# Paired query transposes, alternating GpSimd sums, and the row maximum placed by ScalarE in a one-core attention and soft-MoE kernel

## The chip, the cores and the metric

The kernel runs on one core of a Trainium2 chip. The metric is the device time of one execution in microseconds (us); the median of three runs is given, and one further execution was recorded by the hardware profiler.

## The reference, cut to what matters

Inputs are float32. q, k and v have the shape 4 x 8 x 1152 x 64, so there are 32 heads. Only the first function is touched by the change; the two expert layers behind it stay as they are.

```
q_pool = q.reshape(B, H, S // 2, 2, D).mean(axis=3)          # 576 pooled queries per head
scores = scale * q_pool @ k.T                                # 576 x 1152
scores = scores - max(scores, axis=-1)
attn = exp(scores) / (sum(exp(scores)) + 1e-09)
x = attn @ v                                                 # then two expert layers: soft MoE, then h -> g(h) -> out
```

## The kernel before, in words

Each engine has one instruction stream, written out by hand, and the streams meet only through semaphores. Below, `m` or `n` is a head.

A head is 9 key tiles of 128 keys and 576 queries (4 full tiles of 128, one of 64). Keys stand on the row (partition) side of the scores, so one step of TensorE makes a 128 x 576 piece of scores for one or two key tiles. Both operands are split in a rounded high part and a low part, so that three fast products stand for one precise product. The head dimension is 64, half of the 128 rows, and two products run side by side on the two row halves; for this the queries (`q_hi`, `q_lo`) are wanted twice, on rows 0 to 63 and on rows 64 to 127. A fourth product (`k_one` with `q_neg`) adds minus the row maximum of each query.

What one head takes, by engine:

- SyncE's queue loads `k_raw`, `q_raw`, `v_sb`, takes sums of exponentials through a small transpose by DMA (`turn_sums`), and in heads 4 to 28 loads one 512 KB piece of expert weights.
- GpSimd (POOL): `prepare(m)` adds the two raw queries of each pair into `q_pool`; `divide_x` divides the result of an earlier head by its sums (two instructions, L470 and L473); `head(n)` makes six additions of 128 x 576 tiles into `p_sum` (L487, then L490 five times), each of which waits on a semaphore for the one before it, because all of them add to the same tile.
- ScalarE (ACT): nine `exp_step` of 128 x 576 (L1048); `round_k` and `round_q` (L1062), which copy the turned keys and queries from PSUM into the rounded tiles; `double_q` (L1077), which copies the pooled queries beside themselves, so that the transpose sets each query tile on both row halves; `read_x` (L1057, L1058).
- VectorE (DVE): `tops` finds row maxima over six jobs (L1327, L1321, L1323), `join_tops` joins them (L1334), `place_neg_max` spreads the turned maximum into `q_neg` with one multiplication by the mask `h_mask` (L1341), `low_k`, `low_q`, `low_ends` make the low parts (L1301), `add_pair` adds two probability tiles (L1361).
- TensorE (PE), in this order: nine `scores` steps (L634 to L640) with the six `row_max` jobs of the next head between them (L602, L595, L597); `turn(n + 2, 0)` and `turn(n + 2, 1)`, which transpose the keys (L563), the query tiles (L568, four of them), and the two ends (L571, L573); `turn_neg_max(n + 1)` (L611); `weigh(n)` (L657), the product with v; `add_up(n)` (L668), which sums `p_sum` and the pair over the rows.

The waits that tie a head to the next: `add_up(n)` waits for POOL's sixth addition and for `add_pair(n)`; `row_max(n + 2, 0)` waits for `low_ends(n + 2)`; `scores(n + 1, 0)` waits for `place_neg_max(n + 1)`; each `scores` step waits for the exponential two steps back; POOL's first addition of a head waits for its third exponential, and `add_up` of the head before. Of the tiles, `probs` and `p_sum` exist once.

## Time and profile before

| what | us |
| --- | --- |
| median of 3 runs (lowest, highest) | 748.4 (746.4, 750.25) |
| the profiled execution: time | 750.26 |
| the profiled execution: span from first to last instruction | 748.6 |
| attention part, up to the last `add_up` (us of the span) | 0 to 457 |
| expert layers | 457 to 748.6 |

Times in a row are us from the start of the span. A row of the timeline merges neighbouring instructions of one line, with their count behind the x; "idle before" in brackets is how long the engine had nothing and who released it.

### The profile page before, as it was taken

The numbers are of one execution on the slowest core, as the hardware profiler recorded it, in microseconds if no ns is written. First come the engines' busy times: TensorE is split into PE (matmuls) and PEld (weight loads), VectorE is DVE, ScalarE is ACT, GpSimd is POOL, SyncE is SP. The second block draws the span as 40 slices with busy tenths as digits, with TensorE's granted clock in tenths as the row PEclk, the third lists the DMA queues.
The fourth block names the chain that finished last, engine by engine and source line by source line (L and its number), as shares of the span: only waits on it lengthen the run. The fifth ranks groups of instructions, "written<-read, shape, count | busy, mean of one in ns | idle before, by whom it ended". The sixth has DMA issues, their size and how long they took to land.

```text
span 748.6 us, 16967 instructions
## 1 busy us (share of the span) xinstructions
PE 734.8 (98%) x6439; PEld 549.2 (73%) x6439; DVE 480.2 (64%) x764; ACT 395.4 (53%) x784; POOL 477.8 (64%) x399
## 2 busy tenths in 40 slices
PE   8999999999999999999999999999999999999997
PEld 6776777777777767777777776533678888888886
DVE  7776776776766777767767746523895554554542
ACT  2564665655655646646656543313765454545453
POOL 2588788788787887887887873210784444444442
PEclk9999999999999999999999999999999999999999
DMA  4223434444344344344343218899401010101011
GB/s 117 72 72 85 119 94 134 119 115 128 103 129 127 90 140 118 93 134 119 102 135 109 79 26 300 319 388 370 179 1 43 0 43 1 42 0 42 0 43 42
DMA packets 51621, 81.82 MB, mean 109 GB/s; under 512 B 14556, under 2 KB 20572, under 8 KB 51548
## 3 DMA queue, kind: packets, MB, share of 16 engines
q1 hardware_dynamic: 51468, 80.69, 35.1%
q8 instruction: 49, 0.80, 0.4%
q14 instruction: 24, 0.20, 0.1%
q10 hardware_dynamic: 80, 0.13, 0.0%
HBM read 75.94 MB, written 4.79 MB: 108 GB/s over the span
## 4 chain that ended last, share of the span: by engine, by line
PE 86%; POOL 6%; DVE 4%; issue 3%; ACT 0%; DMA 0%; SPq 0%; POOLq 0%; DVEq 0%; ACTq 0%
PE ps L657 17%; PE ps L963 8%; PE ps L962 8%; PE ps L964 8%; PE ps L634 7%; PE ps L602 6%; PE ps L638 5%; PE ps L636 5%; PE ps L640 4%; POOL p_sum L490 4%; PE ps L668 3%; PE ps L563 2%; PE ps L850 2%; PE ps L952 2%; PE ps L876 2%
## 5 line engine op out<-in xcount | busy, mean ns | idle before, releaser
L490 POOL TENSOR_TENSOR p_sum<-p_sum,probs 128x576 f32<-128x576 f32 x158 | 235.5, 1490 | 23.2 <-ACT probs L1048 0.9
L1327 DVE TENSOR_REDUCE mx<-ps 128x2 f32<-128x1024 f32 (+1 forms) x160 | 189.3, 1218 | 79.9 <-PE ps L602 77.8
L1048 ACT ACTIVATE probs<-ps 128x576 f32<-128x576 f32 x288 | 183.6, 651 | 40.0 <-PE ps L640 26.0
L529 POOL TENSOR_TENSOR g_lo<-g_buf,g_hi 128x384 fp32r<-128x384 f32 x96 | 102.0, 1065 | 99.2 <-ACT g_hi L1214 99.2
L657 PE MATMUL ps<-probs,v_sb 128*64 128x288 f32 x1152 | 146.8, 409 | 0.1
L657 PEld LDWEIGHTS ps<-probs,v_sb 128*64 128x64 f32 x1152 | 79.8, 137 | 56.1 <-issue 5.1
L1562 DVE SCALAR_TENSOR_TENSOR v_buf<-u_buf 128x384 f32<-128x384 f32 x96 | 60.8, 634 | 87.3 <-ACT u_buf L1207 86.3
L962 PE MATMUL ps<-wo_hi,g_hi 128*128 128x512 f32 x282 | 110.5, 392 | 1.1 <-POOL g_lo L529 1.1
L964 PE MATMUL ps<-wo_lo,g_hi 128*128 128x512 f32 x282 | 110.8, 393 | 0.0
L963 PE MATMUL ps<-wo_hi,g_lo 128*128 128x512 f32 x282 | 110.6, 392 | 0.0
L1207 ACT ACTIVATE u_buf<-ps,half 128x384 f32<-128x384 f32 x96 | 55.7, 582 | 92.7 <-PE ps L952 92.7
L634 PE MATMUL ps<-q_hi,k_hi 64*128 64x288 f32 x576 | 101.7, 335 | 0.6 <-DVE q_neg L1341 0.6
L638 PE MATMUL ps<-q_lo,k_hi 64*128 64x288 f32 x576 | 88.8, 292 | 0.0
L636 PE MATMUL ps<-q_hi,k_lo 64*128 64x288 f32 x576 | 88.5, 292 | 0.0
L640 PE MATMUL ps<-q_neg,k_one 64*128 64x288 f32 x576 | 88.4, 290 | 0.0
L1077 ACT ACTIVATE q_pool<-q_pool 128x320 f32<-128x320 f32 x32 | 15.1, 472 | 135.0 <-POOL q_pool L462 134.9
L487 POOL TENSOR_TENSOR p_sum<-probs 128x576 f32<-128x576 f32 x32 | 45.5, 1422 | 56.6 <-issue 48.2
L634 PEld LDWEIGHTS ps<-q_hi,k_hi 64*128 64x128 f32 x576 | 55.7, 184 | 23.9 <-ACT probs L1048 21.7
L602 PE MATMUL ps<-k_hi,q_hi 64*128 64x512 f32 x320 | 70.9, 429 | 0.8 <-DVE mx L1327 0.5
L962 PEld LDWEIGHTS ps<-wo_hi,g_hi 128*128 128x128 f32 x282 | 53.0, 188 | 14.9 <-issue 3.2
L964 PEld LDWEIGHTS ps<-wo_lo,g_hi 128*128 128x128 f32 x282 | 52.9, 188 | 11.6
L636 PEld LDWEIGHTS ps<-q_hi,k_lo 64*128 64x128 f32 x576 | 57.9, 185 | 2.7
(213 smaller groups left out, 1103.0 us busy)
## 6 DMA issues: line engine op xcount, KB each, us to landing
pre<-in_moe_w SPq DMA_DIRECT2D x41, 512.0 KB, 4.6
k_raw<-in_k SPq DMA_DIRECT2D x32, 288.0 KB, 4.0
v_sb<-in_v SPq DMA_DIRECT2D x32, 288.0 KB, 3.4
q_raw<-in_q SPq DMA_DIRECT2D x32, 256.0 KB, 2.5
from_x<-in_moe_w SPq DMA_DIRECT2D x9, 512.0 KB, 5.5
p_inv<-inv_dram SPq DMA_DIRECT2D x62, 72.0 KB, 2.7
out<-o_stage SPq DMA_DIRECT2D x34, 128.0 KB, 2.3
staged<-in_moe_w SPq DMA_DIRECT2D x8, 512.0 KB, 7.9
```

The source lines that it names most:

```text
L490: nc.gpsimd.tensor_tensor(total, total, probs[:, u, :], ALU.add).then_inc(probs_added, 1)
L602: mm = pe.matmul(ps[:, job_bank(m, j) + g, :], q_hi[m % 2][rows_of(g), P * t:P * t + P], k_hi[m % 2][rows_of(g), 0:KP], start=True, stop=True)
L634: mm = pe.matmul(out, k_hi[n % 2][rows, t], q_hi[n % 2][rows, cols], start=True, stop=False)
L636: mm = pe.matmul(out, k_lo[n % 2][rows, t], q_hi[n % 2][rows, cols], start=False, stop=False)
L638: mm = pe.matmul(out, k_hi[n % 2][rows, t], q_lo[n % 2][rows, cols], start=False, stop=False)
L640: mm = pe.matmul(out, k_one[rows, :], q_neg[n % 2][rows, cols], start=False, stop=True)
L657: mm = pe.matmul(ps[D * h:D * h + D, 4, 0:HALF], v_sb[n % 2][:, u, :], probs[:, u, HALF * h:HALF * h + HALF], start=(i == 0), stop=(i == N ...
L962: pe.matmul(o, g_hi[par][:, f, toks], wo_hi[:, f, :], start=(f == 0), stop=False)
L963: pe.matmul(o, g_lo[par][:, f, toks], wo_hi[:, f, :], start=False, stop=False)
L964: mm = pe.matmul(o, g_hi[par][:, f, toks], wo_lo[:, f, :], start=False, stop=(f == NF - 1))
L1048: nc.scalar.activation(dst, ps[:, b0:b0 + 2, 0:HALF], ACT.Exp, scale=SCORE_SCALE).then_inc(exp_done, 1)
L1327: top = nc.vector.tensor_reduce(mx[0:w, NC * t:NC * t + 2], ps[0:w, b:b + 2, :], AX.X, ALU.max)
```

## The change

Three things are done to the attention part. (1) `double_q` is gone. `q_pool` holds the pooled queries once, with a copy of the last tile made by a second small POOL instruction; TensorE transposes two query tiles at a time (two transposes in place of four), which leaves even tiles on rows 0 to 63 and odd tiles on rows 64 to 127 of PSUM bank 7. `round_q` sets each on both row halves with four ScalarE copies of 64 x 256 in place of one of 128 x 512, and `low_q` on VectorE takes four instructions in place of one. The queries are prepared two heads ahead instead of three, and at the head's beginning instead of its end; SyncE's loads follow. (2) POOL's six additions go by turns into `p_sum` and a new tile `p_sum2`, so that most do not wait for the one just before; the sixth adds the two. (3) `place_neg_max` moves from VectorE (one multiplication) to ScalarE (five copies with a 0/1 scale per row, `neg_mask`), and `h_mask` is gone. On VectorE, `add_pair` moves ahead of `low_q` and `low_ends`.

```diff
-                    ("ones", D), ("eps", 1), ("half", 1), ("l_neg", B + 1), ("all_neg", 1),
+                    ("ones", D), ("eps", 1), ("half", 1), ("neg_mask", QT), ("l_neg", B + 1), ("all_neg", 1),
...
-        ROUNDS = 4
+        ROUNDS = 7
...
+        def turned_q(odd):
+            return ps[rows_of(odd), 7, 0:QF // 2 * P].rearrange("r (a c) -> r a c", c=P)
+
+        def by_turns(x, g, odd):
+            return x[rows_of(g), 0:QF * P].rearrange("r (a two c) -> r a two c", two=2, c=P)[:, :, odd, :]
...
             for n in range(HEADS):
-                if n == 0:
-                    load_q(2)
                 if n + 2 < HEADS:
+                    load_q(n + 2)
                     load_k(n + 2)
-                if n + 3 < HEADS:
-                    load_q(n + 3)
...
-                nc.gpsimd.tensor_tensor(q_pool[:, :, 0, :], q_raw[:, :, 0:D], q_raw[:, :, D:2 * D],
+                nc.gpsimd.tensor_tensor(q_pool[:, 0:QT, :], q_raw[:, :, 0:D], q_raw[:, :, D:2 * D], ALU.add)
+                nc.gpsimd.tensor_tensor(q_pool[:, QT, :], q_raw[:, QF, 0:D], q_raw[:, QF, D:2 * D],
                                         ALU.add).then_inc(q_pooled, 1)
...
             def head(n):
-                total = p_sum[:, :]
+                sums = (p_sum[:, :], p_sum2[:, :])
                 if n > 1:
-                    pool.wait_ge(q_pooled, min(n + 3, HEADS))
+                    pool.wait_ge(q_pooled, min(n + 2, HEADS))
                     divide_x(n - 2)
-                for u in range(ADDS if n < HEADS - 1 else LAST_ADDS):
-                    pool.wait_ge(exp_done, NT * n + 3 + u // 2 * 2)
-                    if u == 0:
-                        if n > 0:
-                            pool.wait_ge(sums_done, n)
-                        nc.gpsimd.tensor_tensor(total, probs[:, NT - 1, :], probs[:, 0, :], ALU.add).then_inc(probs_added, 1)
-                    else:
-                        pool.wait_ge(probs_added, ADDS * n + u)
+                if n + 2 < HEADS:
+                    prepare(n + 2)
+                pool.wait_ge(exp_done, NT * n + 3)
+                if n > 0:
+                    pool.wait_ge(sums_done, n)
+                    pool.wait_ge(probs_added, ADDS * n)
+                nc.gpsimd.tensor_tensor(sums[0], probs[:, NT - 1, :], probs[:, 0, :], ALU.add).then_inc(probs_added, 1)
+                pool.wait_ge(exp_done, NT * n + 5)
+                nc.gpsimd.tensor_tensor(sums[1], probs[:, 1, :], probs[:, 2, :], ALU.add).then_inc(probs_added, 1)
+                if n == HEADS - 1:
+                    pool.wait_ge(probs_added, ADDS * n + 1)
+                    nc.gpsimd.tensor_tensor(sums[0], sums[0], probs[:, 3, :], ALU.add).then_inc(probs_added, 1)
+                else:
+                    for u in (3, 4, 5):
+                        pool.wait_ge(exp_done, NT * n + 5 + u // 4 * 2)
+                        pool.wait_ge(probs_added, ADDS * n + u - 2)
+                        total = sums[(u + 1) % 2]
                         nc.gpsimd.tensor_tensor(total, total, probs[:, u, :], ALU.add).then_inc(probs_added, 1)
-                if n + 3 < HEADS:
-                    prepare(n + 3)
+                last = ADDS if n < HEADS - 1 else LAST_ADDS
+                pool.wait_ge(probs_added, ADDS * n + last - 1)
+                nc.gpsimd.tensor_tensor(sums[0], sums[0], sums[1], ALU.add).then_inc(probs_added, 1)
...
-                    pe.wait_ge(q_doubled, m + 1)
-                    for t in range(QF):
-                        pe.transpose(ps[:, 7, P * t:P * t + P], q_pool[:, t, :, :].rearrange("p two d -> p (two d)"), ident[:])
+                    pe.wait_ge(q_pooled, m + 1)
+                    for t in range(QF // 2):
+                        pe.transpose(ps[:, 7, P * t:P * t + P], q_pool[:, 2 * t:2 * t + 2, :].rearrange("p two d -> p (two d)"),
+                                     ident[:])
...
-                high(qh[:, 0:P * QF], ps[:, 7, :])
+                for g in range(2):
+                    for odd in range(2):
+                        high(by_turns(qh, g, odd), turned_q(odd))
...
-            def double_q(m):
-                act.wait_ge(q_pooled, m + 1)
-                nc.scalar.activation(q_pool[:, :, 1, :], q_pool[:, :, 0, :], ACT.Copy).then_inc(q_doubled, 1)
-
+            def place_neg_max(m):
+                act.wait_ge(neg_full, m + 1)
+                r = D + QT
+                for t in range(QT):
+                    last = nc.scalar.activation(q_neg[m % 2][0:r, P * t:P * t + P], ps[0:r, neg_bank(m), 0:P], ACT.Copy,
+                                                scale=neg_mask[0:r, t:t + 1])
+                last.then_inc(neg_free, 1)
...
                 if n + 2 < HEADS:
                     round_k(n + 2)
                     round_q(n + 2)
-                if n + 3 < HEADS:
-                    double_q(n + 3)
+                if n + 1 < HEADS:
+                    place_neg_max(n + 1)
                 if n + 1 < HEADS:
                     read_x(n)
...
             def low_q(m):
-                dve.wait_ge(rounded, ROUNDS * m + 2)
-                low(q_lo[m % 2][:, 0:P * QF], ps[:, 7, :], q_hi[m % 2][:, 0:P * QF])
+                dve.wait_ge(rounded, ROUNDS * m + 5)
+                for g in range(2):
+                    for odd in range(2):
+                        low(by_turns(q_lo[m % 2], g, odd), turned_q(odd), by_turns(q_hi[m % 2], g, odd))
...
                     tops(n + 1, n > 0)
-                    place_neg_max(n + 1)
                 else:
                     invert_sums(n - 1)
                 if n + 2 < HEADS:
                     low_k(n + 2)
-                    low_q(n + 2)
-                    low_ends(n + 2)
                 if n + 1 < HEADS:
                     add_pair(n)
                 else:
                     top_logits(0)
                     add_last(n)
+                if n + 2 < HEADS:
+                    low_q(n + 2)
+                    low_ends(n + 2)
```

## Rows read from the trace of the kernel before

**Rows 1.** The page: busy time by engine, and the chain by engine.
```profile
PE 734.8 (98%) x6439; PEld 549.2 (73%) x6439; DVE 480.2 (64%) x764; ACT 395.4 (53%) x784; POOL 477.8 (64%) x399
...
PE 86%; POOL 6%; DVE 4%; issue 3%; ACT 0%; DMA 0%; SPq 0%; POOLq 0%; DVEq 0%; ACTq 0%
```

**Rows 2.** Timeline, PE: where `weigh` begins in heads 2 and 9 (start, length).
```profile
55.92 0.46 PE L657 MATMUL ps<-probs,v_sb 128*64 128x288 f32 x2
...
151.94 0.46 PE L657 MATMUL ps<-probs,v_sb 128*64 128x288 f32 x2
```

**Rows 3.** Timeline, PE: end of head 21, turns and `weigh` of head 22, next `row_max`.
```profile
321.18 0.41 PE L657 MATMUL ps<-probs,v_sb 128*64 128x288 f32 x2
...
321.53 0.45 PE L668 MATMUL ps<-p_sum,ones 128*32 128x144 f32 x8
...
329.87 0.60 PE L568 MATMUL ps<-ident,q_pool 128*128 128x128 f32 x4
330.31 0.27 PE L571 MATMUL ps<-ident,k_raw 128*128 128x128 f32 x1
...
330.73 4.59 PE L657 MATMUL ps<-probs,v_sb 128*64 128x288 f32 x36
...
335.87 0.53 PE L602 MATMUL ps<-k_hi,q_hi 64*128 64x512 f32 x2
```

**Rows 4.** Timeline, POOL: head 22, up to the first addition of head 23.
```profile
325.58 1.42 POOL L487 TENSOR_TENSOR p_sum<-probs 128x576 f32<-128x576 f32 x1 [1.61 <-issue]
327.15 7.98 POOL L490 TENSOR_TENSOR p_sum<-p_sum,probs 128x576 f32<-128x576 f32 x5
...
333.39 1.74 POOL L490 TENSOR_TENSOR p_sum<-p_sum,probs 128x576 f32<-128x576 f32 x1
...
335.09 0.86 POOL L462 TENSOR_TENSOR q_pool<-q_raw 128x320 f32<-128x320 f32 x1
...
336.92 0.81 POOL L473 TENSOR_TENSOR x_t<-x_raw,p_inv 64x288 f32<-64x288 f32 x1
339.29 1.42 POOL L487 TENSOR_TENSOR p_sum<-probs 128x576 f32<-128x576 f32 x1 [1.57 <-issue]
```

**Rows 5.** Timeline, DVE: the low parts and `add_pair` of head 22.
```profile
332.18 0.68 DVE L1301 TENSOR_TENSOR q_lo<-ps,q_hi 128x512 fp32r<-128x512 f32 x1
332.78 0.28 DVE L1301 TENSOR_TENSOR k_lo<-ps,k_hi 128x128 fp32r<-128x128 f32 x1
...
333.11 0.77 DVE L1361 TENSOR_TENSOR probs<-probs 128x576 f32<-128x576 f32 x1
```

**Rows 6.** Timeline, ACT: fifth exponential, roundings and `double_q` of head 22.
```profile
326.36 0.65 ACT L1048 ACTIVATE probs<-ps 128x576 f32<-128x576 f32 x1 [0.16 <-PE ps L640]
...
330.73 0.60 ACT L1062 ACTIVATE q_hi<-ps 128x512 fp32r<-128x512 f32 x1
331.22 0.27 ACT L1062 ACTIVATE k_hi<-ps 128x128 fp32r<-128x128 f32 x1
...
335.99 0.47 ACT L1077 ACTIVATE q_pool<-q_pool 128x320 f32<-128x320 f32 x1 [4.38 <-POOL q_pool L462]
```

**Rows 7.** Timeline, PE: from `weigh` to the sums in the last head.
```profile
456.44 0.41 PE L657 MATMUL ps<-probs,v_sb 128*64 128x288 f32 x2
456.68 0.66 PE L675 MATMUL ps<-p_sum,ones 128*64 128x288 f32 x4
```

**Rows 8.** Timeline, PE: the same seam in head 10.
```profile
169.58 0.66 PE L657 MATMUL ps<-probs,v_sb 128*64 128x288 f32 x4
...
170.37 0.45 PE L668 MATMUL ps<-p_sum,ones 128*32 128x144 f32 x8
```

**Rows 9.** Timeline, POOL: last addition of head 30.
```profile
443.67 1.40 POOL L490 TENSOR_TENSOR p_sum<-p_sum,probs 128x576 f32<-128x576 f32 x1
```

**Rows 10.** Timeline, PE: the seam behind it in head 30.
```profile
444.35 0.41 PE L657 MATMUL ps<-probs,v_sb 128*64 128x288 f32 x2
445.13 0.45 PE L668 MATMUL ps<-p_sum,ones 128*32 128x144 f32 x8 [0.36 <-POOL p_sum L490]
```

More of the change, by code:

```diff
@@ L161, in soft_moe_chain @@
     ident, phi_sb, mx, half, ones, eps = (small[n] for n in ("ident", "phi_sb", "mx", "half", "ones", "eps"))
-    sum_ident, fold, l_neg, all_neg, row, ref_neg, w_exp, w_last, e_sum, e_mass, e_den, e_inv, c_top, c_sum, c_inv = (
-        small[n] for n in ("sum_ident", "fold", "l_neg", "all_neg", "row", "ref_neg", "w_exp", "w_last", "e_sum", "e_mass",
+    neg_mask, sum_ident, fold, l_neg, all_neg, row, ref_neg, w_exp, w_last, e_sum, e_mass, e_den, e_inv, c_top, c_sum, c_inv = (
+        small[n] for n in ("neg_mask", "sum_ident", "fold", "l_neg", "all_neg", "row", "ref_neg", "w_exp", "w_last", "e_sum", "e_mass",
                            "e_den", "e_inv", "c_top", "c_sum", "c_inv"))
@@ L499, in _ @@
             prepare(1)
-            prepare(2)
             for n in range(HEADS):
@@ L573, in turn @@
                     mm = pe.transpose(ps[:, tail_bank(m), P:2 * P],
-                                      q_pool[:, QF, :, :].rearrange("p two d -> p (two d)"), ident[:])
+                                      q_pool[:, QF:QT + 1, :].rearrange("p two d -> p (two d)"), ident[:])
                 mm.then_inc(turned, 1)
@@ L1070, in round_q @@
                 act.wait_ge(turned, 2 * m + 2)
-                high(qh[:, 0:P * QF], ps[:, 7, :])
+                for g in range(2):
+                    for odd in range(2):
+                        high(by_turns(qh, g, odd), turned_q(odd))
                 high(kh[:, KP:KP + P], ps[:, b, 0:P])
                 high(qh[:, P * QF:SQ], ps[:, b, P:P + QLAST])
-            def double_q(m):
-                act.wait_ge(q_pooled, m + 1)
-                nc.scalar.activation(q_pool[:, :, 1, :], q_pool[:, :, 0, :], ACT.Copy).then_inc(q_doubled, 1)
-            double_q(0)
+            def place_neg_max(m):
[5 more added lines that the diff above has]
+                last.then_inc(neg_free, 1)
             round_k(0)
             round_q(0)
-            double_q(1)
             round_k(1)
             round_q(1)
-            double_q(2)
+            act.wait_ge(consts_ready, 1)
+            place_neg_max(0)
+            act.wait_ge(zeroed, 1)
             for n in range(HEADS):
@@ L1388, in _ @@
             low_ends(1)
-            place_neg_max(0)
-            dve.wait_ge(zeroed, 1)
             low_q(1)
```

21 lines of the change are left out of this document (6 added, 15 removed).

## The prediction

> **What bounds the kernel now.** I read the page first: PE is busy for 98% of the span and makes 86% of the chain of waits, POOL 6% [rows 1]. That says to look at PE, and that POOL comes onto the chain somewhere. All the edits lie in the attention part, so I went to the timeline of that part, engine by engine. The period is steady: `weigh` begins at 55.92 in head 2 and at 151.94 in head 9, so a head takes 96.02 / 7 = 13.72 us [rows 2].
>
> Two loops could set this period, and the whole question is which. The PE loop is everything PE does in a head, with its short waits for exponentials. The POOL loop goes: six additions, `add_up`, the first scores of the next head, three exponentials, and again the first addition. Head 21 shows both at the seam between `weigh` and `add_up`. The last addition of head 22 ends at 333.39 + 1.74 = 335.13, and in head 21 the corresponding one lies as near to its `add_up`. PE starts its last pair of `weigh` products at 321.18 and `add_up` at 321.53, .35 later [rows 3]; within `weigh` pairs are (4.59 - 0.41) / 17 = .25 apart [rows 3]. I find the .35 in 27 of the 31 such seams while POOL's end wanders by some hundredths, so in those POOL isn't what ends the wait, or just not. How near it is, the late heads tell. In head 10 the seam is 170.37 - (169.58 + .24) = .55 [rows 8] (three heads are like it: 10, 17 and 24), and in head 30 it is 445.13 - 444.35 = .78, with POOL named as releaser [rows 9, 10]; there PE starts 445.13 - (443.67 + 1.40) = .06 behind POOL's end. In the regular head it starts about .13 behind it: 335.13 against 335.87 less the .62 that `add_up` takes, 335.25 [rows 3, 4]. So PE's own loop is 13.72 and POOL's is 13.72 - .07 = 13.65. A change of one loop alone gives almost nothing; both have to become shorter.
>
> **Part 1, two transposes fewer on PE.** Four query transposes take 330.31 - 329.87 = .44, .11 each [rows 3], so two fewer give .22 a head. They are on the PE loop if nothing behind them is late: `weigh` would start at 330.51 in place of 330.73. The exponentials are over by then, since ACT starts to round q at 330.73 with the keys' .60 before it [rows 6]. I therefore count the .22 in full for 30 heads: 6.6 us. PE's new loop is 13.50.
>
> What pays for it lies on ACT and DVE. A rounding of 512 columns lasts .60 and the next starts .49 later; one of 128 lasts .27 [rows 6]. A copy of 256 columns so lies between, near .38, at a pace of about .27: four of them take 1.1 in place of .5, and `round_q` ends about .6 later, near 332.0. Five placements of 128 columns at .16 to .27 each take .8 to 1.4, until 333.4 at the latest. The price of a scale read from a tile isn't in this trace; its bounds are that of a plain 128-column copy, .27, and that of 512 columns, .60, which gives 335.0 for the end. I take .27, the same shape. The cover is ACT's idle time of 4.38 before 335.99, which existed because `double_q` waited for POOL [rows 6]. Even the upper bound ends before `read_x` can start, near 336.0. Without that cover all of it would lie ahead of the next exponentials. `double_q`'s .47 goes too, and it lay ahead of the first exponential; but that one also waits for the first scores, which follow `row_max` at 335.87 [rows 3], and by the timeline these end as ACT comes free. I count nothing for it.
>
> On DVE the low part of 512 columns lasts .68 and of 128 .28, so 256 columns come to .41, and .08 of each overlaps with the next (332.18 + .68 against 332.78) [rows 5]: four take 1.33 in place of .60. `place_neg_max` is gone from DVE. `add_pair` now stands ahead of them, and behind it are queued `low_q` and `low_ends`, on which `row_max(n + 2, 0)` waits. The order in time: `low_k` (.68, from about 330.75, when the keys' rounding is over) until 331.4, `add_pair`, then 1.33 + .33 of low parts.
>
> **Part 2, the additions.** Now the second addition starts at 327.15 and the sixth at 333.39, 1.56 apart where one lasts 1.42: a handoff of about .14 each [rows 4]. In the new order the second addition needs the fifth exponential, which ends at 326.36 + .65 = 327.01 [rows 6]; with a handoff it starts at 327.15, as now. Four additions without handoff bring it to 327.15 + 4 x 1.42 = 332.83, the last one depends on its forerunner, 332.97, and takes 1.42. It ends at 334.39 if nothing disturbs it.
>
> Something does: the sixth now takes 1.74 in place of 1.42, beside `add_pair` at 333.11, and `add_pair` lasts .77 [rows 4, 5]. The nearest reading is that one waits for the other. I keep the .32, and the sum ends at 334.71 against 335.13: .42 sooner. Bounds: no disturbance, .74 sooner; a whole `add_pair` of .77 on POOL's row, .03 less than nothing, that is no gain. The middle value stands because in the new order, too, `add_pair` would be held up by an addition under way (331.41 to 332.83) and then collide with one behind a handoff.
> The Trainium skill (SBUF — State Buffer, "Who interferes with whom") says that a VectorE instruction with two SBUF inputs and a GpSimd instruction that reads SBUF exclude each other for the whole instruction. The stretched row agrees with it. The low parts, which read one input from PSUM, would by that rule not disturb POOL however many they are, and the sum by it is the same.
>
> POOL's loop so becomes 13.65 - .42 = 13.23, under PE's 13.50 by .27. `prepare` and its second small instruction (between nothing and the .86 of the large one, I take .3) move ahead of the first addition: 337.73, where `divide_x` ends now [rows 4], plus .3, with `divide_x` and `prepare` only changing places. That leaves over 1 us before 339.29, and at worst .7. The loads change places on SyncE: the query load stands ahead of the key load, and both wait for turns that are past. The queries are needed by `prepare` some 5 us later. I count nothing. If a load came late by more than about 1 us, POOL's first addition would be late.
>
> **Part 3, the late heads.** Where POOL was late, its .42 pays besides. Heads 10, 17 and 24: .55 - .35 = .20 each, .6 in all [rows 3, 8]. Head 30: .78 - .35 = .43, of which .4 [rows 3, 10].
>
> **The start.** Both first turns come before the loops. Four roundings and four low parts in place of one each stand there uncovered: .6 + .7, less the four transposes saved. Part of it lies beside `tops`, which bounds the start. Bounds 0 and 1.3; I take .3 against.
>
> **The sum.** 6.6 + .6 + .4 - .3 = 7.3 us. Against the profiled execution, 750.26 (span 748.6 and 1.7 around it), that gives 743.0. The median of the runs is 1.9 lower, and I forecast 748.4 - 7.3 = 741.1. A measurement of this kernel tells about .5%, 3.7 us, from no change.
>
> **Rivals.**
>
> *POOL stays the bound.* `add_pair` now meets additions that follow each other with no gap, and if additions back to back are themselves slower than 1.42, the .42 goes. For it: .32 is lost today with a handoff to hide part of it. Against it: .27 of slack. If nothing at all is gained on POOL, the period is 13.65, 30 x .07 = 2.1 us, no late head is mended, and the time is 746.6 with the start's .3. Half of the gain gives about 743.5. Chance .17, with one third of it inside .5%.
>
> *DVE's queue is late (slower than before).* `low_q` and `low_ends` must be done when `row_max` is due, in the new period at 335.87 - .22 = 335.65. DVE is held until 332.83 by the addition under way, `add_pair` ends near 333.45 and the low parts near 335.1: .55 to spare. If a piece on 64 rows costs as much as the full instruction does, .60, they end at 333.45 + 4 x .60 + .33 = 336.18, .53 late each head. Less the .22 that is .31 x 30 = 9.3: 757 with the loss at the start. The same comes about if `add_pair` doesn't get in between two additions and waits for the one gap left, behind the fifth. It decides once DVE needs more than 2.2 from the end of `add_pair`'s wait plus its own .6. For it: no 64-row form of this instruction with 256 columns is in the trace. Against: cost goes with the columns in every pair of rows that I have [rows 5]. Chance .10.
>
> *The seam closes (more gain).* With the sums early, `add_up` could follow `weigh` without the extra .10. In the last head the products behind `weigh` follow at 456.68 - 456.44 = .24, with all their inputs long there [rows 7]. If .35 was due to a late POOL, each head gains .11 x 30 = 3.3 more: 737.8. Against it: in the last head the products keep the shape 128 x 64, whereas `add_up` changes to 128 x 32, and the .35 doesn't vary with POOL. Chance .12.
> The Trainium skill (TensorEngine Tiling (Array Packing), "Key Properties") has it that a change of tiling mode drains TensorE. By it the .10 stays and the forecast holds; the two seams fit it and don't prove it [rows 3, 7].
>
> *The forecast* keeps .61.
>
> **How the numbers follow.** The likeliest case gives 741.1, and its own range is 739.0 to 743.5, from the bounds of the start and the scatter of the runs. Over all cases the range goes from the closed seam to POOL nearly unchanged, 737.5 to 746.0, which leaves out the slow case and a little at both ends. Faster by more than .5% (under 744.7): .61 + .12 + two thirds of .17 = .84, less .03 for the scatter, .81. Within .5%: the rest of POOL's case and some of DVE's, .10. Slower .09.
>
> **What the profile of the changed kernel would show.** `weigh` to `weigh` 13.50. L568's successor with two transposes a head and `weigh` starting .22 sooner behind the last scores. Last pair of `weigh` to `add_up` .35 in every head (.24 if the seam closes, more with POOL named if POOL bounds). Additions 1.42 apart, one stretched. `low_ends` done .5 before `row_max`; if not, PE idles there with DVE named. ACT idle again, over 2 us, before `read_x`. Wrong would make me, above all, an addition that isn't 1.42 when back to back, and a DVE piece dearer than .41.

## The result and the profile after

The changed kernel takes 743.5 us (median of 5 runs, 742.75 to 743.81), the kernel before 747.9 beside it (5 runs, 746.4 to 750.25). The ratio is 0.9934, 95% interval 0.9916 to 0.9951: by it the change saves 4.9 us of the 747.9, between 3.7 and 6.3; the medians by themselves differ by 4.4. The forecast was 741.1, with a range of 737.5 to 746.0. The profiled execution of the changed kernel took 742.75 with a span of 741.1, 7.5 less than that of before, so one pair of executions gives more than the medians do; the next section says why.

The page of the changed kernel, busy time and the chain by engine:

```profile
PE 724.7 (98%) x6375; PEld 540.8 (73%) x6375; DVE 524.0 (71%) x826; ACT 456.2 (62%) x1008; POOL 485.5 (66%) x431
...
PE 91%; DVE 5%; POOL 1%; issue 1%; ACT 1%; DMA 0%; SPq 0%; DVEq 0%; ACTq 0%
```

Against [rows 1] PE has 10 us less, ACT 61 more, DVE 44 more, and POOL went from 6% of the chain to 1%. The work that ACT and DVE took over lies beside PE's work in the heads. The timeline of PE in head 21, from the query transposes to the next row maximum:

```profile
312.30 0.38 PE L581 MATMUL ps<-ident,q_pool 128*128 128x128 f32 x2
312.52 0.27 PE L585 MATMUL ps<-ident,k_raw 128*128 128x128 f32 x1
312.63 0.27 PE L587 MATMUL ps<-ident,q_pool 128*128 128x128 f32 x1
312.74 0.27 PE L625 MATMUL ps<-ident,neg_max 128*128 128x128 f32 x1
312.94 4.59 PE L671 MATMUL ps<-probs,v_sb 128*64 128x288 f32 x36
317.46 0.45 PE L682 MATMUL ps<-p_sum,ones 128*32 128x144 f32 x8
...
318.09 0.50 PE L616 MATMUL ps<-k_hi,q_hi 64*128 64x512 f32 x2
```

Two transposes take .22 where four took .44 [rows 3], and `weigh` follows at once. From here to `weigh` of head 22, at 326.42, are 13.48 us, against 13.72 before [rows 2]. POOL in the same head:

```profile
307.95 1.43 POOL L492 TENSOR_TENSOR p_sum<-probs 128x576 f32<-128x576 f32 x1 [1.42 <-ACT probs L1062]
309.51 1.43 POOL L494 TENSOR_TENSOR p_sum<-probs 128x576 f32<-128x576 f32 x1
310.90 4.16 POOL L503 TENSOR_TENSOR p_sum<-p_sum,probs 128x576 f32<-128x576 f32 x3
315.13 1.81 POOL L506 TENSOR_TENSOR p_sum<-p_sum,p_sum 128x576 f32<-128x576 f32 x1
317.11 0.80 POOL L474 TENSOR_TENSOR x_t<-x_raw,p_inv 64x288 f32<-64x288 f32 x1 [0.17 <-POOL p_sum L506]
317.98 0.80 POOL L477 TENSOR_TENSOR x_t<-x_raw,p_inv 64x288 f32<-64x288 f32 x1
318.86 0.88 POOL L465 TENSOR_TENSOR q_pool<-q_raw 128x320 f32<-128x320 f32 x1
```

The additions run from 307.95 to 316.94, 8.99 us against 9.55 [rows 4]; the last one is stretched to 1.81 (1.74 before). POOL now ends .52 before `add_up` (317.46), where it ended .13 before. DVE and ACT beside it:

```profile
313.13 0.69 DVE L1318 TENSOR_TENSOR k_lo<-ps,k_hi 128x512 fp32r<-128x512 f32 x1 [1.00 <-ACT k_hi L1076]
313.77 1.90 DVE L1373 TENSOR_TENSOR probs<-probs 128x576 f32<-128x576 f32 x1
315.59 1.72 DVE L1318 TENSOR_TENSOR q_lo<-ps,q_hi 64x256 fp32r<-64x256 f32 x4
317.33 0.29 DVE L1318 TENSOR_TENSOR k_lo<-ps,k_hi 128x128 fp32r<-128x128 f32 x1
317.54 0.21 DVE L1318 TENSOR_TENSOR q_lo<-ps,q_hi 128x64 fp32r<-128x64 f32 x1
```

```profile
312.50 0.60 ACT L1076 ACTIVATE k_hi<-ps 128x512 fp32r<-128x512 f32 x1
313.00 1.58 ACT L1076 ACTIVATE q_hi<-ps 64x256 fp32r<-64x256 f32 x4
314.60 0.28 ACT L1076 ACTIVATE k_hi<-ps 128x128 fp32r<-128x128 f32 x1
314.77 0.22 ACT L1076 ACTIVATE q_hi<-ps 128x64 fp32r<-128x64 f32 x1
314.88 1.38 ACT L1095 ACTIVATE q_neg<-ps,neg_mask 69x128 fp32r<-69x128 f32 x5
318.31 0.41 ACT L1071 ACTIVATE x_raw<-ps 128x288 f32<-128x288 f32 x1 [2.05 <-PE ps L682]
```

The row of `add_pair` begins at 313.77 and ends at 315.67. That is 1.90 us where it takes .77 in [rows 5], so I read it as waiting for the addition that ran until 315.06. POOL's last addition begins at 315.13 by its row, but it ends at 316.94; less the usual 1.42 that is 315.52, when `add_pair` was nearly done. `low_ends` is over at 317.75, .34 before the row maximum at 318.09. ACT is idle for 2.05 us before it copies the sums out.

### The profile page after: what moved, and what is told of

It is laid out like the page before. It is cut to its first block, busy times and chain, and to the rows that moved or that the text cites. A ratio compares the mean times of both kernels' runs of the same rounds, so it can differ in the third digit from the quotient of the medians.

```text
span 741.1 us, 17095 instructions
## 1 busy us (share of the span) xinstructions
PE 724.7 (98%) x6375; PEld 540.8 (73%) x6375; DVE 524.0 (71%) x826; ACT 456.2 (62%) x1008; POOL 485.5 (66%) x431
## 4 chain that ended last, share of the span: by engine, by line
PE 91%; DVE 5%; POOL 1%; issue 1%; ACT 1%; DMA 0%; SPq 0%; DVEq 0%; ACTq 0%
PE ps L671 20%; PE ps L648 8%; PE ps L977 8%; PE ps L978 8%; PE ps L976 8%; PE ps L616 6%; PE ps L650 5%; PE ps L652 5%; PE ps L654 5%; PE ps L682 3%; PE ps L576 3%; PE ps L890 2%; PE ps L966 2%; PE ps L864 2%; DVE v_buf L1572 1%
## 5 line engine op out<-in xcount | busy, mean ns | idle before, releaser
L503 POOL TENSOR_TENSOR p_sum<-p_sum,probs 128x576 f32<-128x576 f32 x93 | 129.2, 1416 | 0.0
L1318 DVE TENSOR_TENSOR q_lo<-ps,q_hi 64x256 fp32r<-64x256 f32 (+1 forms) x160 | 60.5, 379 | 2.0 <-ACT q_hi L1076 0.7
```

The lines of the kernel that those rows point to most:

```text
L503: nc.gpsimd.tensor_tensor(total, total, probs[:, u, :], ALU.add).then_inc(probs_added, 1)
```

## Where the profiled executions stand to the medians

To compare kernels I take two marks from each trace: the start of the first product of `add_up` in head 0 and in head 30. They cut the span into a start, thirty heads, and the rest.

| kernel | start, to the sums of head 0 | heads 0 to 30 | rest | span |
| --- | --- | --- | --- | --- |
| before | 32.97 | 412.16 | 303.4 | 748.6 |
| before, again | 33.02 | 411.88 | 303.5 | 748.4 |
| changed | 34.26 | 404.25 | 302.6 | 741.1 |
| changed, again | 36.15 | 404.19 | 303.6 | 743.9 |

The heads repeat within .3 us. The start and the rest don't, and both go with TensorE's granted clock, which has two levels, full and half. In the first profile of the changed kernel the record has the lower level from 12.9 to 19.8 us, in the second from 13.4 to 27.1, and there also from 477.6 to 481.0, a stretch in which the first one kept the full clock. Every trace of this study with such a low stretch between 470 and 486 us has 303.4 us or more for the rest (nine traces), every one without it 302.6 to 302.8 (four). Three rows of the windows view (busy time by engine, then granted clock, DMA share and GB/s), first of the changed kernel and then of its second run:

```profile
12.00:20.00 8.00, 6.37 (x29) 4.78 (x29) 6.53 (x14) 3.75 (x12) 1.93 (x4) 0.57 0.38 107
```

```profile
12.00:27.00 15.00, 13.06 (x75) 10.71 (x75) 12.13 (x20) 6.34 (x16) 3.41 (x5) 0.55 0.28 83
470.00:485.00 15.00, 13.71 (x104) 5.97 (x106) 6.78 (x21) 2.52 (x6) 4.61 (x4) 0.89 0.86 324
```

So of the 7.4 us between the first two spans, 7.9 are the heads, -1.3 the start, and .8 the rest. I put the .8 to the clock and not to the change: four of the nine traces with the paired transposes lack the low stretch, and the kernel before has executions whose mean granted clock is 1.000 (746.41 and 746.54 us in its second run), in which it can't lie either.

The -1.3 isn't what the change costs at the start, because the two kernels began at different clocks. The view gives 1.00 for the first microseconds of every trace, but the pace of like instructions shows the level. Five products with `ident`, which only keep PE busy, in the kernel before, in the kernel before with alternating sums (the run `e2_sums_only` below) and in the changed kernel:

```profile
7.61 1.27 PE L705 MATMUL ps<-ident 128*128 128x128 f32 x5
```

```profile
6.60 0.71 PE L715 MATMUL ps<-ident 128*128 128x128 f32 x5
```

```profile
6.59 0.71 PE L719 MATMUL ps<-ident 128*128 128x128 f32 x5
```

That is (1.27 - .42) / 4 = .21 from one to the next in the first, the pace also of the low stretches on record, and .11 in the others. Both profiles of the kernel before ran at the slow pace until 11 us, the changed kernel until 6.1. A fair pair is the changed kernel and `e2_sums_only`: fast from 6.1 and 5.3 us on, then 6.8 us at the lower level in each, and neither has VectorE's work on `h_mask` (which in the kernel before is over at 5.2, two microseconds ahead of VectorE's next instruction, and so isn't what delays it).

| start of | row maxima on DVE | first scores | sums of head 0 | lower level on record |
| --- | --- | --- | --- | --- |
| before | 9.65 | 19.11 | 32.97 | 14.4 to 17.9 |
| sums only | 8.05 | 17.62 | 31.62 | 12.1 to 18.9 |
| sums, `add_pair` moved | 8.24 | 17.64 | 31.49 | 12.8 to 16.3 |
| changed | 10.19 | 20.27 | 34.26 | 12.9 to 19.8 |
| changed, one chain | 10.04 | 20.11 | 34.97 | 12.2 to 19.1, 22.5 to 25.9 |

At like clocks the start of the changed kernel is 34.26 - 31.62 = 2.6 us longer (2.5 at the first scores, 20.11 less 17.62, if the run with one chain stands for it, whose pace agrees best), twice what the profiles of before suggest. The table also shows what the clock costs: between 12 and 19 us 3.4 us more of the lower level cost next to nothing (31.62 against 31.49), but beyond 20, where PE is busy, 3.4 us at the lower level cost .9 (from the first scores to the sums, 14.86 against 13.99), and 7.3 us cost 1.7 in the second profile of the changed kernel.

## The experiments

**The kernel before, again.**

> The kernel before, unchanged, run and profiled a second time. The five times of the kernel before spread over 3.9 us (746.4 to 750.25) and those of the changed kernel over 1.1 (742.75 to 743.81), and the two profiled executions differ by 7.5 us where the medians differ by 4.4. Theory A (the profiled execution of before was a slow one in its attention part, by late heads): a second profile shows fewer or other late heads, a first-to-last distance of the sums of heads 0 and 30 below 412.16 us by up to 1, and the same period of 13.72. Rival B (the scatter lies behind the heads, in the stretch where expert weights are streamed): heads 0 to 30 again take 412.2 within 0.3, and the 303.4 us behind them differ by 1 or more. Either way the ratio to the kernel before is 1.000 within 0.002.

Measured: ratio 0.9998 (0.9984 to 1.0012), 12 runs of 746.4 to 750.1. Heads 411.88, with the same late heads 10, 17, 24 and 30; start 33.02, rest 303.5. Neither theory is borne out: the second profile repeats the first in all three parts, late heads included. At 750.1 it stands, like the first at 750.3, above the median of its kernel, so both say too much for what a typical execution of before takes.

What makes a head late can be read in both traces. In heads 10, 17 and 24 one single step on POOL takes .3 longer than in all others: the first addition starts .43 behind the third exponential in place of .13, or the second or the third starts .43 behind the end of the one before in place of .14. In head 10:

```profile
160.79 1.42 POOL L487 TENSOR_TENSOR p_sum<-probs 128x576 f32<-128x576 f32 x1 [1.89 <-issue]
```

The usual idle time there is 1.57 [rows 4]. Why the step is longer, no run shows. Head 30 has no such step. There POOL's loop shows because PE's is shorter: no head 32 is left for it to turn.

**The alternating sums alone.**

```diff
-    h_mask = at("h_mask", [P, QT, P], M)
+    p_sum2 = at("p_sum2", [P, SQ], M)
...
-                total = p_sum[:, :]
+                sums = (p_sum[:, :], p_sum2[:, :])
...
+                        total = sums[(u + 1) % 2]
...
-                                        h_mask[0:r, :, :], ALU.mult).then_inc(neg_free, 1)
+                                        neg_mask[0:r, :].unsqueeze(2).to_broadcast([r, QT, P]), ALU.mult).then_inc(neg_free, 1)
```

> The kernel before with the alternating sums alone; four transposes, one rounding, maximum on VectorE as before. (The mask is read as a broadcast 128 x 5 tile, since the second sum takes its place.) Theory (PE's loop is the bound, POOL's had 0.07 us to spare): the period stays 13.72, POOL ends its additions 0.4 to 0.5 us before the sums in place of 0.13, the late heads 10, 17, 24 and 30 are mended, heads 0 to 30 take 411.1 in place of 412.2, and the time falls by 1.1 us: ratio 0.9985. Rival (POOL was the bound, and its gain is what the changed kernel lives on): the period falls to 13.4, 10 us less, ratio 0.987.

Measured: 747.6, ratio 0.9988 (0.9976 to 0.9999). Period 13.71, no late heads, heads 410.95 against 412.16 and 411.88. The size is the theory's. Its picture of POOL was wrong: first to last addition still took 9.56 us, and POOL ended .13 before the sums, as before. POOL, then DVE:

```profile
315.62 1.41 POOL L497 TENSOR_TENSOR p_sum<-p_sum,probs 128x576 f32<-128x576 f32 x1
317.10 2.43 POOL L500 TENSOR_TENSOR p_sum<-p_sum,p_sum 128x576 f32<-128x576 f32 x1
```

```profile
317.39 0.21 DVE L1308 TENSOR_TENSOR q_lo<-ps,q_hi 128x64 fp32r<-128x64 f32 x1
317.52 0.74 DVE L1368 TENSOR_TENSOR probs<-probs 128x576 f32<-128x576 f32 x1
```

The four additions in the middle came 1.37 apart, but the last, begun at 317.10, took 2.43 us, though `add_pair` began .42 later than it. What the alternation won, the collision took. POOL's end now hangs on `add_pair`'s: it lies .134 before the sums in every head. The long step of the late heads isn't in this trace at all, nor in that of the changed kernel; why, stays open.

**The chain of sums put back into the changed kernel.**

```diff
-                sums = (p_sum[:, :], p_sum2[:, :])
+                total = p_sum[:, :]
...
+                for u in range(ADDS if n < HEADS - 1 else LAST_ADDS):
+                    pool.wait_ge(exp_done, NT * n + 3 + u // 2 * 2)
...
+                        pool.wait_ge(probs_added, ADDS * n + u)
```

> The changed kernel with its six additions put back into one chain on one tile; everything else as changed. Theory (two loops side by side): POOL's loop of 13.58 to 13.65 is now the bound, PE waits for POOL before the sums in every head (seam 0.43 to 0.50 in place of 0.34), late heads come back; heads 0 to 30 take 404.25 + 30 x 0.1 to 0.17 + 1, that is 408 to 410, and the time is 4 to 6 us above the changed kernel. Rival (the sums do nothing here, all of the gain is the transposes): heads 0 to 30 take 404.3 and the time is that of the changed kernel within 0.5.

Measured: 747.8, ratio 0.9989 (0.9978 to 1.0), 3.8 to 4.3 us above the changed kernel's medians. Period 13.567, seam .41 in the regular heads (PE idle, POOL named, 15.6 us in 30 places over 60 to 430 us), POOL .053 before the sums; heads 407.64. That is the theory, a little below its lower edges (.43 for the seam, 408 for the heads, 4 us for the time). Late heads came back: 9 and 29, each with one step of .43 or .44 on POOL, and 30.

**add_pair moved, in the kernel before with alternating sums.**

```diff
                     low_k(n + 2)
-                    low_q(n + 2)
-                    low_ends(n + 2)
                 if n + 1 < HEADS:
                     add_pair(n)
...
+                if n + 2 < HEADS:
+                    low_q(n + 2)
+                    low_ends(n + 2)
```

> The kernel before with the alternating sums, as in the run e2_sums_only, and add_pair moved ahead of low_q and low_ends. Theory (alternating sums end sooner only if add_pair does not begin beside the last addition): first to last addition 9.0 us in place of 9.56, POOL ends .5 before the sums and add_pair waits for the fifth addition, as in the changed kernel; yet the period stays 13.71, since TensorE's own loop is as long as before; heads 0 to 30 take 411.0, time that of e2_sums_only within 0.7. Rival A (POOL did hold something up): period below 13.68. Rival B (the collision has another cause): the last addition again takes 2.4.

Measured: 747.4, ratio 0.9991 (0.9981 to 1.0001). First to last addition 8.93, POOL ends .75 before the sums, and the period is 13.72, heads 410.93. The last addition took 1.81. POOL's loop is now well below PE's, and it is worth nothing: PE's own loop is shown to be 13.72. (The theory had .5 for the .75; rival A and rival B are out.)

**add_pair moved back, in the changed kernel.**

> The changed kernel with add_pair back behind low_q and low_ends on VectorE. In the run e2_sums_only the alternating sums ended no sooner than one chain does (9.56 us from first to last addition, as before), because the last addition took 2.43 us: it began at 317.10, add_pair at 317.52, and it ended 1.42 minus .15 behind the end of add_pair. Theory (an addition that VectorE's add_pair overtakes within its first .4 us waits for all of it): here add_pair would begin 1.6 us behind the last addition, which is then undisturbed, 1.41; POOL ends .9 before the sums; but add_pair itself ends only about when the sums are due, so PE now waits for VectorE: period 13.49 to 13.60, time 0 to 4 us above the changed kernel, add_pair named as what the sums wait for. Rival (the collision does not depend on where add_pair stands): the last addition takes 1.8 or more as now.

Measured: 749.0, ratio 1.0006 (0.9995 to 1.0016): all of the gain is gone, more than the 4 us that the theory allowed. Period 13.609, seam .46; heads 407.88, 3.6 more than the changed kernel. The start takes 36.48 to the sums of head 0, of which .7 is that head's own wait; this profile was at the slow pace until 24.5 us, so the other 1.5 can't be put to the order of `add_pair`. POOL, DVE and PE:

```profile
306.26 1.41 POOL L506 TENSOR_TENSOR p_sum<-p_sum,p_sum 128x576 f32<-128x576 f32 x1
307.85 1.38 POOL L474 TENSOR_TENSOR x_t<-x_raw,p_inv 64x288 f32<-64x288 f32 x1 [0.17 <-POOL p_sum L506]
```

```profile
305.73 1.73 DVE L1318 TENSOR_TENSOR q_lo<-ps,q_hi 64x256 fp32r<-64x256 f32 x4 [0.78 <-ACT q_hi L1076]
...
307.81 0.75 DVE L1373 TENSOR_TENSOR probs<-probs 128x576 f32<-128x576 f32 x1
```

```profile
307.52 1.14 PE L671 MATMUL ps<-probs,v_sb 128*64 128x288 f32 x8
308.71 0.33 PE L682 MATMUL ps<-p_sum,ones 128*32 128x144 f32 x4
```

The last addition is undisturbed, 1.41, and POOL is done 1.04 before the sums. `add_pair` ends at 308.56, and PE goes on at 308.71. Now `add_pair` collides with `divide_x` instead (1.38 in place of .80). With four pieces of `low_q` ahead of it, and these held .78 for ACT's roundings, `add_pair` is what the sums wait for; the profile names no releaser here, and the reading rests on the two times. The move of `add_pair` is thus a necessary part of the change.

**The maximum placed by VectorE, in the changed kernel.**

```diff
-                for t in range(QT):
-                    last = nc.scalar.activation(q_neg[m % 2][0:r, P * t:P * t + P], ps[0:r, neg_bank(m), 0:P], ACT.Copy,
-                                                scale=neg_mask[0:r, t:t + 1])
...
+                nc.vector.tensor_tensor(q_neg[m % 2][0:r, :].rearrange("r (t c) -> r t c", t=QT),
+                                        ps[0:r, neg_bank(m), 0:P].unsqueeze(1).to_broadcast([r, QT, P]),
+                                        neg_mask[0:r, :].unsqueeze(2).to_broadcast([r, QT, P]), ALU.mult).then_inc(neg_free, 1)
...
             low_ends(1)
+            place_neg_max(0)
+            dve.wait_ge(zeroed, 1)
             low_q(1)
             low_k(1)
```

> The changed kernel with the placement of the row maximum back on VectorE, as one multiplication of 69 x 640 (the mask is read as a broadcast tile of five columns). ScalarE is free of five copies, 1.38 us a head. Theory (neither place is on a loop; add_pair waits for POOL's fifth addition anyway): low_k starts .8 later, add_pair still ends where it does, the period stays 13.485 within .02, ScalarE is idle 3.4 us in place of 2.05 before it copies out the sums; at the start the first scores come earlier by up to .7, since ScalarE's placement stood behind four roundings. Time within 1 us of 743.4, rather below. Rival (the move to ScalarE is a part of the gain): the period rises by .1 or more, over 3 us in all.

Measured: 746.6, ratio 0.9965 (0.9951 to 0.998), 3.1 us above the changed kernel, and this I missed. Yet the period is 13.488, POOL ends .53 before the sums, and ACT is idle 3.3 to 3.8 us: in the heads the theory holds (404.81, of which .5 is one late head). The rival has the time right, over 3 us, and the mechanism wrong, since the period didn't rise. The loss lies in the start, 36.94, and in the rest, 304.6. At the start the clock was low until 20.95 and again from 24.4 to 27.8. Against the run with `add_pair` moved back, which like this one ran at the slow pace until 20 us and more, the first scores come no sooner (21.28 against 21.32), and the second head's row maximum comes .8 later (23.42 against 22.65):

```profile
23.42 0.50 PE L616 MATMUL ps<-k_hi,q_hi 64*128 64x512 f32 x2 [1.35 <-DVE k_lo L1305]
```

On VectorE the placement, .81, now stands ahead of the second head's low parts, and that is the .8. In the rest PE waited 2.0 us for one load of expert weights (`w_in`), for which it waits .9 to 1.2 in seven other profiles with the paired transposes. Whether the placement has to do with that wait no run tells. So in this profile .8 is the placement's and .5 the late head's; how much of the 3.1 us between the medians is the placement and how much the clock stays open, with 9 runs that spread from 743.95 to 748.0.

**The same shape on both sides of the seam.**

```diff
-                        for c in range(4):
-                            mm = pe.matmul(ps[SLOTS * c:SLOTS * c + SLOTS, 4, HALF:HALF + QUAD], ones[:, 0:SLOTS],
+                        for c in (0, 2):
+                            mm = pe.matmul(ps[SLOTS * c:SLOTS * c + D, 4, HALF:HALF + QUAD], ones[:, :],
```

> The changed kernel with add_up made of four products of the shape 128 x 64 in place of sixteen of 128 x 32: it sums only two of the four column quarters, twice over, so half of the sums are left out. The seam from the last pair of weigh to add_up is 0.336 in the kernel before and in the changed one, whether POOL ends .13 or .52 before it. Theory (the change of shape on TensorE costs the .09 beyond the pace within weigh, .242): with the same shape on both sides the seam is .24 in every head, and the next one, to the row maxima, stays. Rival (the wait for POOL and VectorE, though over, keeps the weights from being loaded early): the seam stays .33.

Measured (one execution, 740.7 us; half of the sums are left out):

```profile
301.57 0.66 PE L671 MATMUL ps<-probs,v_sb 128*64 128x288 f32 x4
302.05 0.41 PE L682 MATMUL ps<-p_sum,ones 128*64 128x144 f32 x4
```

The last pair of `weigh` starts .24 after 301.57, at 301.81, and the sums .24 behind it, in heads 0 to 29. The waits are the same, so the .10 of the seam belongs to the change of shape. The period is 13.33, .15 less: the .10, and .05 for the products that are left out.

**The start: keys first.**

```diff
-                    pe.wait_ge(turn_free, 3)
+                    pe.wait_ge(turn_free, 4)
...
             low_ends(0)
+            low_k(1)
+            low_q(1)
             low_ends(1)
-            low_q(1)
-            low_k(1)
```

> The changed kernel with one reordering at the start: on VectorE the low part of head 1's keys goes before its queries' low parts and ends (it stood last), and the first scores wait for all of them. VectorE sat idle 1.31 us there, from 17.5 to 18.8. Theory (the start's loss of 1.3 us lies in the pieces of rounding and low parts in front of the first scores and of the second row maximum): the second head's first row maximum, now at 21.60, comes at 20.9 to 21.0, and everything behind it 0.6 to 0.7 sooner, the sums of head 0 at 33.6 in place of 34.26; time about 0.7 below the changed kernel, which the runs can hardly tell. Rival (the start is bound by the first exponentials and the maximum's placement): the sums of head 0 stay at 34.2 to 34.3.

Measured: 743.35, ratio 0.9925 (0.9909 to 0.9941). The sums of head 0 came at 34.99, not 33.6, the first scores at 21.81 and the second head's row maximum right behind them at 22.41. The slow pace lasted until 20.6 there, so the sums of head 0 don't tell the theories apart. Against the run with `add_pair` moved back, which has the changed kernel's order here and as slow a pace, the first scores come .5 later and the second head's row maximum .2 sooner: the order gains a third of what the theory had.

**The start: by halves.**

```diff
-                for g in range(2):
-                    for odd in range(2):
+                for odd in range(2):
+                    for g in range(2):
                         high(by_turns(qh, g, odd), turned_q(odd))
...
-                dve.wait_ge(rounded, ROUNDS * m + 5)
-                for g in range(2):
-                    for odd in range(2):
+                for odd in range(2):
+                    dve.wait_ge(rounded, ROUNDS * m + 3 + 2 * odd)
+                    for g in range(2):
```

> The changed kernel with the reordering of the run e4_start and one thing more: the four rounding copies and the four low parts of the queries go by the PSUM half that they read (both copies of the even tiles, then both of the odd ones), and VectorE starts on the first half when that is rounded, not when all four are. e4_start left the sums of head 0 at 34.99, later than the 34.26 of the changed kernel, but its low granted clock lasted until 20.6 and theirs from 12.9 to 19.8, so that starts can't be compared without the clock. Theory (the start's loss is the pieces in front of the row maxima and of the first scores): the first row maximum on VectorE, at 10.19 in the changed kernel, comes near 9.35, the first scores near 19.4 in place of 20.27 at the same clock, the second head's first row maximum right behind; sums of head 0 at 32.7 (up to 1.5 more where the low clock lasts longer); the heads 404.3 as before; time 1.0 to 1.5 below 743.4. Rival (the clock alone makes the start, the order nothing): sums of head 0 at 34.3 to 35.0, time 743.4.

> The changed kernel, unchanged, on the same chip and in the same rounds as the two runs below. Between calls the median of the kernel before was 747.9 (5 runs), 748.9 (29) and 748.8 (20), so the first ratio, 0.9934, rested on the lowest of them. Theory: heads 0 to 30 again 404.3, median 743.0 to 744.0, ratio 0.992 to 0.994. Rival (the first result was a lucky one, as its start and the stretch of the experts' weights at full clock suggest): median above 744.5.

> The kernel of the run e5_start_halves once more, beside the changed kernel. There its median was 742.8 and the changed kernel's in another call 743.5. Theory (the start gains a part of what it lost): 0.5 to 1.0 us below the changed kernel of this call. Rival (the granted clock makes the start, and the order is nothing beside it): the two agree within 0.4.

Measured: 742.8 in the first run, ratio 0.9926 (0.9912 to 0.9939); in the second 742.0, ratio 0.9922 (0.9905 to 0.9939), beside 743.9 for the changed kernel, ratio 0.9942 (0.9926 to 0.9959). The changed kernel repeats itself as its theory has it: median 743.9, heads 404.19. The sums of head 0 came at 34.29 and 33.08, so by that number the first run sides with its rival. But it ran at the slow pace until 12.8 us, and the second only until 5.1:

| start of | slow pace until | row maxima on DVE | first scores |
| --- | --- | --- | --- |
| changed, one chain | 5.4 | 10.04 | 20.11 |
| by halves, second run | 5.1 | 9.02 | 18.92 |
| changed, `add_pair` moved back | 24.5 | 10.75 | 21.32 |
| by halves, first run | 12.8 | 10.10 | 20.19 |

At the same pace the row maxima come 1.0 sooner and the first scores 1.2 sooner, so the theory's 9.35 and 19.4 are met when the clock is the same; the theory of the pieces is borne out at the start. The version saves 5.8 us against the kernel before (4.6 to 7.1), the most of the study. Over the changed kernel it gains 1.9 by the medians measured beside each other, more than the 0.5 to 1.0 of the theory, but the intervals of the two ratios overlap; its heads are the same (404.28 and 404.12).

## Why the prediction was right, and what was off

**PE's loop and POOL's side by side: shown.** The two parts, alone and together, give for heads 0 to 30: neither 412.2 and 411.9, sums alone 411.0, all but the sums 407.6, both 404.2. The sums are worth 1.1 by themselves and 3.4 behind the transposes. The run with all but the sums has `add_pair` moved and the placement on ScalarE too; the placement changes nothing in the heads (13.488 with it on VectorE), `add_pair`'s place was tried with both sums and found needed, and the two transposes entirely by themselves were not run. Forecast were 13.72 for PE's loop and 13.65 for POOL's; the run with one chain has 13.57 for POOL's, for the most part since its first addition now follows the third exponential by .08 where it took .13.

**Two transposes, 6.6 us: right.** The period fell by .23, from 13.717 to 13.485, forecast 13.50. The cover held: ACT idle 2.05.

**The late heads, 1.0 us: right in sum** (heads 10, 17, 24 and 30 are regular; 412.16 - 404.25 = 7.9 in all, forecast 7.6), but in part by luck. I counted on POOL's new slack of .4 to cover a step that is .3 longer. In the profile of the changed kernel no such step occurs, so the cover was never tried there; in the run with the placement on VectorE a first addition that came .7 late cost head 20 half a microsecond.

**The additions: the size right, the lower bound too high.** 8.99 against the 9.13 of the forecast, whose bounds were 8.81 and 9.58. Additions back to back come 1.37 apart and not 1.42, so the undisturbed six take 8.60, as the run with `add_pair` moved back shows. The collision was read rightly as one instruction waiting for the other. The stretched rows, 1.81, 1.74 and 2.43 us for an addition of 1.42, agree with the Trainium skill's rule (SBUF — State Buffer, "Who interferes with whom") that one of the two fully blocks. That page lets the one that issues first go first. By the recorded starts it isn't so in the run with the sums alone: the addition began at 317.10 and waited for an `add_pair` that began at 317.52. Either a GpSimd addition takes hold of its operands some .4 us after its recorded start, or the order is decided otherwise; the runs don't tell.

**The rivals.** POOL as the bound came only where the chain was put back. The rival had it that half of POOL's gain gives about 743.5; by the prediction's own numbers half of it, .21, still puts POOL's loop (13.44) under PE's 13.50 and costs nothing in the regular heads, so that the measured 743.5 is the same figure is chance. DVE too late for the row maximum came nowhere; too late with `add_pair`, for the sums, it came where `add_pair` was put back. In the changed kernel .34 were to spare, forecast .55, because a piece of 64 x 256 takes .42 and the next starts .43 later, where I had let them overlap. The seam didn't close: it is .336 in the changed kernel with POOL .52 ahead, and .24 only where the shape is the same. The Trainium skill's sentence (TensorEngine Tiling (Array Packing), "Key Properties") that changing the tiling mode drains TensorE agrees with that run.

**The start, .3 us: the step that failed.** It was put as "bounds 0 and 1.3; I take .3 against". At like clocks it is 2.6, outside both bounds. Two things were wrong in it. First the pieces were too cheap: four roundings take 1.57 in place of .60, .97 more where .6 was counted, and four low parts 1.73 in place of .68, 1.05 more where .7 was counted. Second, nothing of them lies beside `tops` in the first turn. The row maxima wait for the roundings, and DVE does the low parts ahead of them, so that all of it delays them: 8.05 became 10.19. The run with the sums alone, then the changed kernel, first ACT, then DVE:

```profile
6.80 0.60 ACT L1072 ACTIVATE q_hi<-ps 128x512 fp32r<-128x512 f32 x1
```

```profile
6.85 1.57 ACT L1076 ACTIVATE q_hi<-ps 64x256 fp32r<-64x256 f32 x4
```

```profile
7.46 0.68 DVE L1308 TENSOR_TENSOR q_lo<-ps,q_hi 128x512 fp32r<-128x512 f32 x1
8.05 4.60 DVE L1334 TENSOR_REDUCE mx<-ps 128x2 f32<-128x1024 f32 x4
```

```profile
8.45 1.73 DVE L1318 TENSOR_TENSOR q_lo<-ps,q_hi 64x256 fp32r<-64x256 f32 x4 [0.71 <-ACT q_hi L1076]
10.19 4.62 DVE L1346 TENSOR_REDUCE mx<-ps 128x2 f32<-128x1024 f32 x4
```

The other .5 comes in the second turn, where the first scores wait for a placement that on ACT stands behind four roundings:

```profile
16.75 1.59 ACT L1076 ACTIVATE q_hi<-ps 64x256 fp32r<-64x256 f32 x4 [3.55 <-PE ps L587]
...
18.64 1.38 ACT L1095 ACTIVATE q_neg<-ps,neg_mask 69x128 fp32r<-69x128 f32 x5
```

The scores begin at 20.27 against 17.62. On top comes the clock: PE waits more at the start, and in eight of the nine traces with the paired transposes the low clock still stands or comes back beyond 20 us, in the four traces without them never. That the waits cause it is argued, not shown.

**The median.** 7.3 were forecast; 4.9 were measured by the first ratio and 4.3 by the second (4.4 and 4.1 by the medians). With 2.6 for the start the same sum gives 6.6 + .6 + .4 - 2.6 = 5.0. It also closes between two kernels whose starts had like clocks: from the sums alone to the changed kernel the heads give 6.7 and the start takes 2.6, which leaves 4.1, and the medians, 747.6 and 743.5 from different sets of runs, are 4.1 apart. The profiles of before, against which I made the sum, lie above its medians by 1.1 to 2.4, of which the slow pace of their first 11 us is about 1.4. That is why the gain between profiles (7.5, 4.5) scatters about that between medians.

## What to carry to other kernels

Where two loops of nearly the same length share a period, price a change by both: here one part was worth 1.1 us alone and 3.4 beside the other. An addition that collides with another engine's isn't made sooner by starting it sooner; look at where the other one starts, and move that. Count the start by itself: pieces that are covered in the steady loop stand bare there. And before two starts are compared, look at the pace of like instructions in each; here a slow first 11 us in one kernel's profiles hid half of what the change costs.

## What was unexpected of the hardware

- A GpSimd addition of 128 x 576 (1.42 us) took 2.43 when VectorE's addition of two SBUF tiles began .42 after it, and 1.81 when that one was under way at its start.
- ScalarE copies of 64 x 256 from PSUM last .38 each and start .40 apart; the copy of 128 x 512 lasts .60 and lets the next start after .49. Copies of 69 x 128 with a scale per row last .37 and start .25 apart. VectorE's subtraction of 64 x 256 lasts .42 and starts .43 apart; that of 128 x 512 lasts .68 and lets the next start after .60.
- A change from 128 x 64 to 128 x 32 products costs TensorE .10 us (.336 against .236).
- A kernel's identical start differed by 1.9 us between two profiles (34.26 and 36.15), with the lower clock from 12.9 to 19.8 and from 13.4 to 27.1.
- Where the record of the granted clock had not begun, the view gave 1.00 though TensorE ran at the slow pace: 128 x 128 products with `ident` came .21 apart in the kernel before at 7.61, and .11 apart in `e2_sums_only` at 6.60.
- In the kernel before, one step of POOL in heads 10, 17 and 24 took .43 us where the others take .13 or .14, in both profiles.
